# Attention, Fourier mixing and two MLPs on one core: the zeroth feature in four runs of small products, low parts of the down weights earlier on VectorE, and the first attention unit's rows by parity

## The reference: what is computed

```python
for b in range(nb):                       # attention, by blocks
    intra = einsum(qb, kb) * Dmask; intra = einsum(intra, vb)
    inter = einsum(qb * lam_pow, kv_state)
    out[:, :, sl] = intra + inter
    kv_state = lam_block * kv_state + einsum(kb * rev_pow, vb)
X = fft(fft(x, axis=1), axis=2)           # x: attention's rows, (2, 768, 512)
u = x + real(X)
y = u + relu(normalised(u) @ w_ch1) @ w_ch2          # first MLP
out = y + relu(normalised(y) * g_ln @ w3) @ w4       # second MLP
```

## Time and profile before

| | us |
|---|---|
| median of 3 runs | 584.24 (583.93 to 588.41) |
| the profiled execution, device time | 584.5 |
| its span, first to last instruction | 582.5 |
| PE busy in it | 568.9 (98%) |
| DVE, ACT, POOL busy | 353.3, 242.7, 162.7 |

### The profile page before, as it was taken

One profiled execution on the slowest core, in us unless ns is written; L12 is line 12 of the kernel. 1 busy time (PEld: TensorE's weight loads), 2 busy tenths in 40 slices (PEclk: granted clock), 3 DMA queues, 4 the chain that ended last, 5 costly groups with the idle time before them and its releaser, 6 DMA issues.

```text
span 582.5 us, 10727 instructions
## 1 busy us (share of the span) xinstructions
PE 568.9 (98%) x4037; PEld 390.6 (67%) x4037; DVE 353.3 (61%) x627; ACT 242.7 (42%) x475; POOL 162.7 (28%) x143
## 2 busy tenths in 40 slices
PE   8999999999899999999999999899999999999997
PEld 4889978666566666666666666566666666666663
DVE  3437788998875775646878676674265433422223
ACT  1255567546663234323546554363222342323231
POOL 1568931763710011003286312620003400000000
PEclk9999999999999999999999999999999999999999
DMA  7999981000137436531235522132000123100001
GB/s 239 393 378 377 351 264 55 2 20 0 37 56 193 132 111 154 136 91 38 74 90 113 141 74 73 36 55 55 19 2 2 37 55 109 73 2 1 0 1 72
DMA packets 78515, 59.85 MB, mean 103 GB/s; under 512 B 39418, under 2 KB 65666, under 8 KB 77060
## 3 DMA queue, kind: packets, MB, share of 16 engines
q1 hardware_dynamic: 76260, 54.49, 32.3%
q10 hardware_dynamic: 1728, 3.15, 1.4%
q0 software_dynamic: 480, 1.57, 0.9%
HBM read 43.73 MB, written 6.30 MB: 86 GB/s over the span
## 4 chain that ended last, share of the span: by engine, by line
PE 77%; DVE 9%; DMA 5%; issue 5%; POOL 3%; ACT 1%; DVEq 0%; SPq 0%; ACTq 0%; POOLq 0%
PE bank L667 36%; PE bank L647 32%; DMA arena<-attn 4%; PE bank L527 2%; PE bank L478 2%; DVE arena L1306 1%; DVE arena L1151 1%; PE bank L473 1%; DVE arena L1149 1%; POOL arena L1479 1%; DVE arena L1158 1%; PE bank L443 1%; PE bank L456 1%; PE bank L591 1%; DVE arena L1271 1%
## 5 line engine op out<-in xcount | busy, mean ns | idle before, releaser
L667 PE MATMUL bank<-arena 128*128 128x512 f16 x1152 | 287.2, 379 | 3.2 <-DVE arena L1158 3.1
L647 PE MATMUL bank<-arena 128*128 128x256 f16 x2016 | 259.3, 273 | 2.7 <-issue 1.9
L647 PEld LDWEIGHTS bank<-arena 128*128 128x128 f16 x2016 | 196.4, 98 | 78.0 <-issue 3.8
L667 PEld LDWEIGHTS bank<-arena 128*128 128x128 f16 x1152 | 112.2, 98 | 90.4 <-DVE arena L1158 3.9
L1306 DVE SCALAR_TENSOR_TENSOR arena<-arena 128x512 f16<-128x512 f32 x96 | 74.2, 773 | 62.4 <-ACT arena L915 62.2
L915 ACT ACTIVATE arena<-arena 128x512 f16<-128x512 f32 x96 | 60.4, 629 | 98.3 <-DVE arena L1353 92.9
L1347 DVE SCALAR_TENSOR_TENSOR arena<-bank,arena 128x256 f32<-128x256 f32 x48 | 20.3, 422 | 65.1 <-PE bank L647 64.7
L1537 POOL TENSOR_TENSOR arena<-arena 128x512 f32<-128x512 f32 x12 | 18.6, 1570 | 90.0 <-DVE arena L1271 90.0
L960 ACT ACTIVATE arena<-bank 128x256 f32<-128x256 f32 x48 | 18.3, 381 | 52.8 <-PE bank L647 52.7
L1283 DVE TENSOR_TENSOR arena<-arena 128x512 f16<-128x512 f32 x42 | 33.0, 796 | 10.1 <-ACT arena L899 10.1
L1353 DVE SCALAR_TENSOR_TENSOR arena<-bank,arena 128x256 f32<-128x256 f32 x48 | 20.2, 421 | 27.4 <-PE bank L647 27.4
(11 more groups left out here) (108 smaller groups left out, 527.1 us busy)
## 6 DMA issues: line engine op xcount, KB each, us to landing
arena<-w SPq DMA_DIRECT2D x48, 256.0 KB, 4.3
arena<-w SPq DMA_DIRECT2D x24, 512.0 KB, 4.5
arena<-attn SPq DMA_DIRECT2D x10, 1024.0 KB, 8.9
out<-arena SPq DMA_DIRECT2D x12, 256.0 KB, 2.3
arena<-attn SPq DMA_DIRECT2D x4, 512.0 KB, 4.2
x_near<-arena ACTq DMA_DIRECT2D x6, 256.0 KB, 7.5
x_far<-arena ACTq DMA_DIRECT2D x6, 256.0 KB, 6.2
arena<-c SPq DMA_DIRECT2D x1, 1153.5 KB, 12.1
```

The source lines that it names most:

```text
L647: last = nc.tensor.matmul(bank_, wst[:, i, wx, w, kt, :], xs[s % 2][:, x, ux, :, kt, :], start=not started and k == 0, stop=k == 5, skip_g ...
L667: last = nc.tensor.matmul(ops[t][:], hT[n % 2][:, half, hx, t * P:(t + 1) * P], wdn[:, i, wx, half * DM:(half + 1) * DM], start=first and ...
```

## The change

1. **Zeroth feature.** The two batches' columns go through one product of 4 moving columns in place of two of 2; the columns of `C1` are stored in another order (all cosines, then all sines) so that one product of 128 stationary columns spans both parities. 15 small products that stood one behind each product of groups 3 to 7 become 12, in four runs of three, behind the whole groups 3, 4, 5 and 7. ACT copies the result out in four instructions instead of two.
2. **Down weights' low parts.** In stage 0 `down_lo(0, i)` is issued before the statistics, `normalise` and `x_lo` of that pair.
3. **Normalising.** In stages 1 to 5 all four tiles are normalised in one go, ahead of the weights' low parts.
4. **First attention unit.** A semaphore for each parity of the mask; `kcol` is copied by ACT instead of DVE; of the first block PE runs the rows of both batches first, each parity as its mask is done, and then `keys_values(0, 0)`. Three products of zeros fewer.
5. **High part of the second up chunk.** On ACT its first half is made ahead of `y_columns(5)` and waits for the first batch's rows to be stored alone (`x_out[0]`); its second half waits for `x_out[1]`, and so does DVE ahead of `up_lo(0, 1)`.

The core of the diff:

```diff
-WARM_BEFORE, WARM_BETWEEN = 11, 24
+WARM_BEFORE, WARM_BETWEEN = 11, 21
-ZEROTH = ((0, 1, 129, 0, 128, 0), (1, 64, 192, 0, 128, 2), (0, 129, 193, 0, 64, 4), (1, 0, 64, 64, 128, 4),
-          (0, 0, 1, 0, 1, 6))
+ZEROTH = {3: (1, 129, 0), 4: (257, 385, 4), 5: (129, 257, 8), 7: (0, 1, 12)}
...
+                if first:
+                    for par in range(2):
+                        pe.wait_ge(mask_done, 2 * u + 1 + par)
+                        for pair in range(PAIRS):
+                            last = values(pair, par)
...
             pe.wait_ge(v_first, 16)
             rows(0, 0, 0, True)
+            rows(0, 1, 0, True)
             keys_values(0, 0, 0, True)
-            rows(0, 1, 0, True)
...
+            def zeroth_feature(f):
+
+                lo, hi, at = ZEROTH[f]
+                for c in range(HALF):
+                    if f == 3 and c == HALF - 1:
+                        pe.wait_ge(sf_done, B * HALF)
+                    column = zeroth_rows if c == 0 else sfold[(HALF + c) % 2][:, :, :, 0].rearrange("p b q -> p q b")
+                    last = nc.tensor.matmul(bank[7][0:hi - lo, at:4 + at], C1[:, c, lo:hi], column,
+                                            start=c == 0, stop=c == HALF - 1)
+                if f == 7:
+                    last.then_inc(zeroth_done, 1)
...
                     for c in range(HALF):
                         last = along(f, c)
-                        if f == 3 and c == HALF - 1:
-                            pe.wait_ge(sf_done, B * HALF)
-                        if f < 8:
-                            zeroth = zeroth_feature(f - 3, c)
                     last.then_inc(f1_done, 1)
-                    if f == 7:
-                        zeroth.then_inc(zeroth_done, 1)
+                    if f in ZEROTH:
+                        zeroth_feature(f)
...
             up_hi(0, 0)
             y_columns(4)
+            act.wait_ge(x_out[0], 16)
+            up_hi(0, 1, (0,))
             y_columns(5)
             y_columns(6)
-            for b in range(B):
-                act.wait_ge(x_out[b], 16)
-            up_hi(0, 1, (0,))
             y_columns(7)
             zeroth_columns()
+            act.wait_ge(x_out[1], 16)
             up_hi(0, 1, (1,))
...
+                if s == 0:
+                    down_lo(0, i)
                 if prep is not None:
...
                     if i == late + 2:
                         row_scale(prep)
-                        normalise(prep, (0, 1))
+                        normalise(prep, range(NT) if s > 0 else (0, 1))
                     for k in X_SECOND[late].get(i, ()):
                         x_lo(prep, k)
-                if s == 0:
-                    down_lo(0, i)
...
                 if prep is not None:
-                    if i == late + 2:
+                    if i == late + 2 and s == 0:
                         normalise(prep, (2, 3))
...
+            dve.wait_ge(x_out[1], 16)
             up_lo(0, 1)
```

More of the change, by code:

```diff
@@ L212, in build @@
                          for name in ("near", "far"))
-        lam_in, pow_step, pow_out, mask_in = sem("lam_in"), sem("pow_step"), sem("pow_out"), sem("mask_in")
+        lam_in, pow_step, pow_out = sem("lam_in"), sem("pow_step"), sem("pow_out")
+        mask_in = [sem(f"mask_in{par}") for par in range(2)]
         powrow_in = sem("powrow_in")
@@ L469, in rows, with values @@
                     pe.wait_ge(x_done, u - 1)
-                pe.wait_ge(mask_done, 2 * u + 2)
-                for pair in range(PAIRS):
-                    if not first:
+                def values(pair, par):
+                    h = 2 * pair + par
+                    v = blk_in[slot].rearrange("p a (b r) n -> p a b (r n)", b=B)[:, 3, b, h * D:(h + 1) * D]
+                    return nc.tensor.matmul(xps[b][:, h * D:(h + 1) * D], PT[b][:, par, pair, :], v,
+                                            start=first, stop=True, skip_group_check=not first)
+                if first:
[3 more added lines that the diff above has]
+                            last = values(pair, par)
+                else:
+                    pe.wait_ge(mask_done, 2 * u + 2)
+                    for pair in range(PAIRS):
                         nc.tensor.matmul(xps[b][:, pair * P:(pair + 1) * P], qd[slot][:, b * PAIRS + pair, :],
                                          state[b][:, pair, :], start=True, stop=True)
-                    for par in range(2):
-                        h = 2 * pair + par
-                        v = blk_in[slot].rearrange("p a (b r) n -> p a b (r n)", b=B)[:, 3, b, h * D:(h + 1) * D]
-                        last = nc.tensor.matmul(xps[b][:, h * D:(h + 1) * D], PT[b][:, par, pair, :], v,
-                                                start=first, stop=True, skip_group_check=not first)
+                        for par in range(2):
+                            last = values(pair, par)
                 last.then_inc(pv_done, 1)
@@ L524, in along @@
                 n = SIN if sin else COS[par]
-                at = par * NE + sin * COS[par]
+                at = (NE + SIN * par) if sin else COS[0] * par
                 lhs = fold[:, b, 2 * par + sin, c, dc * P:(dc + 1) * P]
@@ L543, in first_sequence @@
                 spread_back(0, 1)
-            def zeroth_feature(k, c):
-                par, lo, hi, first, end, at = ZEROTH[k]
-                return nc.tensor.matmul(bank[7][first:end, at:2 + at], C1[:, c, par * NE + lo:par * NE + hi],
-                                        zeroth_rows[:, par, :] if c == 0 else sfold[(HALF + c) % 2][:, :, par, 0],
-                                        start=c == 0, stop=c == HALF - 1)
+            def zeroth_feature(f):
[8 more added lines that the diff above has]
+                    last.then_inc(zeroth_done, 1)
             def sequence(groups):
@@ L753, in _ @@
             nc.scalar.activation(sd[0:1, 0:1], powers[0:1, P - 1:P], ACT.Sqrt)
+            for par in range(2):
+                act.wait_ge(mask_in[par], 16)
+                last = nc.scalar.activation(kcol.rearrange("p (a r) -> p a r", r=2)[:, :, par], DT[:, par, :, 0], ACT.Copy)
+            last.then_inc(kcol_done, 1)
             def x_rows(u):
@@ L852, in zeroth_columns @@
                 act.wait_ge(zeroth_done, 1)
-                nc.scalar.activation(zeroth[:, 0:6], bank[7][:, 0:6], ACT.Copy)
-                nc.scalar.activation(zeroth[0:1, 6:8], bank[7][0:1, 6:8], ACT.Copy).then_inc(zeroth_out, 1)
+                nc.scalar.activation(zeroth[:, 0:4].rearrange("p (t b) -> p t b", t=2),
+                                     bank[7][:, 0:12].rearrange("p (t b) -> p t b", t=2)[:, :, 0:2], ACT.Copy)
+                for par in range(2):
+                    r = slice(64 * par, 64 * par + 64)
+                    nc.scalar.activation(zeroth[r, 4:6], bank[7][r, 8 + 2 * par:10 + 2 * par], ACT.Copy)
+                nc.scalar.activation(zeroth[0:1, 6:8], bank[7][0:1, 12:14], ACT.Copy).then_inc(zeroth_out, 1)
             def middle_out():
@@ L1020, in _ @@
                 n, steps = 2 * n, steps + 1
-            dve.wait_ge(mask_in, 32)
-            for par in range(2):
-                last = nc.vector.tensor_copy(kcol.rearrange("p (a r) -> p a r", r=2)[:, :, par], DT[:, par, :, 0])
-            last.then_inc(kcol_done, 1)
             def masks(u):
@@ L1033, in masks @@
                 for par in range(2):
+                    if u == 0:
+                        dve.wait_ge(mask_in[par], 16)
                     nc.vector.tensor_tensor(PT[b][:, par, :, :], scores[b][par][:].rearrange("p (a n) -> p a n", a=PAIRS),
@@ L1638, in fourier_constants @@
     low, high = 2 * np.arange(P), 256 + 2 * np.arange(64)
-    cols = []
+    cos, sin = [np.cos(2 * np.pi * s[:, None] * (S // 2) / S)], []
     for par in range(2):
```

9 lines of the change are left out of this document (4 added, 5 removed).

## The result

The changed kernel takes **593.65 us** (median of 4 runs, 589.83 to 596.79) against 584.82 for the kernel before, measured beside it (4 runs, 583.93 to 588.41): 1.0139 times as long, 95% interval 1.0075 to 1.0204. The forecast was 578.1, the range 575.3 to 582.0. The profiled execution took 594.65 us, with a span of 592.6. The four runs differ by TensorE's granted clock: at a mean of 0.991, 0.987, 0.983 and 0.979 they take 589.8, 592.7, 594.7 and 596.8 us.

The account below looks back on a forecast made before the run. PE was taken as the bound, busy 568.9 of 582.5 us. Savings of 2.4 + 2.3 + 1.5 + 0.2 = 6.4 us from the profiled 584.5 gave 578.1 us, range 575.3 to 582.0.

Parts of the forecast that it names:

- Part 1: Fourier part: regrouped small products let features(0) start 2.4 us earlier, bounds 1.4 and 3.7.
- Part 5's cover: Fourier part: the second batch's rows land at 73.4, before DVE reaches its new wait at about 75.2.
- Part 2: Stage 0: earlier down_lo saves 0, 0.5 and 1.8 us on PE's three waits, sum 2.3, bounds 0 and 3.1.
- rival A: Stage 0: DVE stays the bound, down_lo waits reappear on sums or square roots; 580.2 us, chance 0.2.
- Part 3: Pairs 26 to 28: the 1.94 us wait goes, a 0.5 us hidden_lo wait comes; 1.5 us saved.
- The bound: Part 3's lower bound: 0.5 us saved if POOL and DVE slow each other for longer.
- Part 4: First attention unit: masks' wait goes, third block's load some 1.3 us earlier; 0.2 us saved, bounds -0.5 and 1.0.
- Rival D: Attention stage, about 20 us: PE stops 1.8 us, clock may fall to 1.2 GHz; likely case 590, chance 0.03.

Follow-up runs that it names:

- no234: Kernel before with only the zeroth feature's four runs and ACT's earlier high part of the second up chunk: 582.33 us, ratio 0.9958.
- early: no34 with all four tiles normalised in one go and splits of the second MLP's weights moved out of pairs 18 and 26: 579.63 us, ratio 0.9915.
- no34: Changed kernel with the one-go normalising and the first attention unit's edit both undone: 581.35 us, ratio 0.9948 to the kernel before.
- no3_fill: Changed kernel with the one-go normalising undone and 32 small unread products added ahead of the attention loop over blocks: 582.75 us, ratio 0.9985.
- the first four experiments: Changed kernel without the one-go normalising, without the first unit's edit, without both; kernel before with that normalising alone: 586.93, 588.47, 581.35, 591.23 us.

## Why the prediction was wrong

**Part 1 held.** Forecast 2.4 us, measured 2.4, by the profile and by `no234`. A run of three full-size small products costs 77.97 - 77.38 = 0.59 us (forecast 0.66), the run of the three one-column products 0.29 (forecast 0.6); the saving could not be more, for PE still waits 0.29 for ACT's copy. `features(0)` starts at 80.68, which less the attention's 4.5 is the forecast 76.2, and `turn` at 94.93, which is the forecast 90.4. That it fits so well is partly luck: the runs cost less than taken, and a wait was left that was forecast to go. Part 5's cover held too: DVE has no idle time ahead of its new wait.

**Part 2 had the right mechanism in two pairs and too large a size.** 2.3 us forecast, 0.6 by the profile, 1.0 by `no234`. The wait of pair 3 went to ACT's copy as the working said, but grew from 0.81 to 1.25 us, and the other two all but went (0.15 left). What the term left out was a new wait of 1.15 us in pair 6, where `down_lo` itself comes late: 3.1 less 1.25, 0.15 and 1.15 is the 0.6. The work of pair 5 on DVE and POOL, after, and then before:

```profile
159.43 1.75 DVE L1321 SCALAR_TENSOR_TENSOR arena<-arena 128x512 f16<-128x512 f32 x1
161.11 2.28 DVE L1173 SCALAR_TENSOR_TENSOR arena<-arena 128x1024 f16<-128x1024 f32 x1
...
158.65 1.98 POOL L1569 TENSOR_TENSOR arena<-arena 128x512 f32<-128x512 f32 x1
160.59 1.71 POOL L1572 TENSOR_TENSOR arena<-arena 128x512 f32<-128x512 f32 x1
```

```profile
159.30 0.68 DVE L1306 SCALAR_TENSOR_TENSOR arena<-arena 128x512 f16<-128x512 f32 x1
160.50 1.27 DVE L1158 SCALAR_TENSOR_TENSOR arena<-arena 128x1024 f16<-128x1024 f32 x1
...
160.66 2.24 POOL L1560 TENSOR_TENSOR arena<-arena 128x512 f32<-128x512 f32 x1 [3.29 <-DVE arena L1283]
```

Before, POOL stood still for 3.29 us until 160.66. Now it still works, for its run of sums from 146.25 on took 16.1 us (before, from 143.68 on, 13.7) beside a DVE that no longer pauses, and `hidden_lo` and `down_lo` take 4.0 us instead of 2.0. So the gain went to the same contention that undid part 3. It is near rival A (DVE stays the bound), in part, though A looked for it on a sum or on a square root.

**Part 3 is one of the two failed steps.** The gain was real: the 1.94 us wait went, and `early`, which keeps it, is 1.7 us under `no34`. The price failed: "what stood in between is 1.0 us later (two tiles, 0.99)". It came 4.9 us later, beside the 5.1 us by which pair 27 starts later anyway. The 0.99 was measured where the two tiles ran before POOL began. Moved ahead, tiles 1 to 3 run beside POOL, which also has no pause now, so the four take 3.83 where two took 1.0 before, 2.8 of the 4.9 us. `down_lo` and `hidden_lo` behind them are stretched as well (2.28 for 1.27, 1.74 for 0.68 before), 1.0 and 1.1 more; `up_lo` was stretched already before. The low part of the hidden half ends at 382.4, 4.4 us after PE wants it, where 0.5 was forecast. The bound named this contention and charged 1 us for it once, though it applies to every instruction that stands beside POOL's. And pair 18, with the same pattern, was dismissed with "or PE has no wait there; nothing": it had no wait before, and got one of 2.2.

**Part 4 is the other.** +0.2 us forecast, 5.6 lost. The sum for it argued that the stage is DMA's, at 0.99, so that PE's idle time there costs nothing. That holds only while PE runs at full clock. At half clock, PE became the bound of the stage, and DMA had nothing left to do at 34 us; with the clock kept up by fillers (`no3_fill`) 4.2 of the 5.6 came back. Rival D had the place (20 us) and the mechanism, with 1.8 us of idle time, for which it took the clock's survival of 1.94 us elsewhere as evidence against. The idle time was 2.8 to 3.5, because block 1 landed 1.0 to 2.5 us later than before, which nothing in the working had moved and whose cause stays open. It was given 0.03; the working itself counted on an idle stretch as long as any in the trace of before, and no row told what a longer one does, so that was too low. Its price of 590 was too high for one such fall: 10 us at half clock cost 4.2.

## What to carry over

Before an edit that removes short waits of TensorE, look at what idle time they leave in one piece: several waits of half a microsecond can be free where one of three microseconds costs four more through the clock. Where that stretch can't be avoided, a few products that nothing reads, put ahead of the wait, are cheap, though not complete, insurance. Price an instruction that is moved by the rows of its new neighbours: work of VectorE that came to stand beside GpSimd's cost about double here, and so did all that followed it there.

## What the runs showed of the hardware

In the profiled executions TensorE's granted clock fell to half with idle stretches of 2.8, 3.2, 3.5 and 4.4 us, and not with those of 1.2, 1.7 and 1.9 us; with one of 2.2 us it fell in one profile and not in two others. In the three profiles with a stretch of 4.4 us it fell 2.5 to 3.3 us into it, with 2.8 to 3.5 us within 0.2 us of its end, and with the 2.2 us 1.3 us behind its end. It stayed down for 3.4, 6.8 or 10.2 us, though TensorE was busy without a pause once the wait was over. Runs without a profile show low mean clocks too, even one of the 17 of the kernel before beside the first four experiments (0.991, 587.85 us); which idle stretches those had is not on record. I had taken one survived wait of 1.94 us as a sign that waits don't matter to it. Of VectorE, beside GpSimd at work: `tensor_scalar` on a 128 x 512 float32 tile 0.96 us against 0.48, the 128 x 1024 low part 2.28 against 1.27, the 128 x 512 one 1.74 against 0.69.
